# Mask tables of a block-causal attention in float32r in place of bf16

## The reference

```python
scores = scale * np.matmul(q, k.transpose(0, 1, 3, 2))
mask = block_i >= block_j            # block = position // 64
scores = np.where(mask, scores, -1000000000.0)
attn = softmax(scores)               # written out with its maximum and its sum
x = np.matmul(attn, v)               # then laid out as 2304 tokens x 512
h = x @ w_in;  x = (h * clip(h + 3, 0, 6) / 6) @ w_out       # 512 -> 2048 -> 512
h = x @ w_in2; out = (h * tanh(log1p(exp(h)))) @ w_out2      # 512 -> 2048 -> 512
```

## Time and profile before

| | |
|---|---|
| median of 3 runs | 1002.57 us (1001.17 to 1003.04) |
| profiled execution, its own time | 1002.3 us |
| span of the profiled execution | 1000.5 us |
| busy share of TensorE, VectorE, ScalarE, GpSimd | 97%, 76%, 65%, 52% |
| TensorE clock granted | full speed in all 40 slices |
| attention | from the start to about 212 us |
| masks | 128 matmuls of 64 columns, 8.9 to 206.3 us |

### The profile page before, as it was taken

How to read it: one execution, slowest core, us unless ns; L and a number is a source line. 1 busy time by engine, 2 the same in 40 slices (tenths; PEclk the granted TensorE clock), 3 DMA queues, 4 the chain that set the end, 5 groups by cost and what they waited for, 6 DMA issues and landing times.

```text
span 1000.5 us, 17885 instructions
## 1 busy us (share of the span) xinstructions
PE 966.3 (97%) x6132; PEld 857.7 (86%) x6132; DVE 764.5 (76%) x1231; ACT 645.5 (65%) x1429; POOL 523.5 (52%) x493
## 2 busy tenths in 40 slices
PE   6999999999999999999999999999999999999998
PEld 5887888899988888988888999888898988889896
DVE  5998888878687766769797776877868887776654
ACT  6888888855455444545546456777777767776663
POOL 7888899967766586957776671221212222010000
PEclk9999999999999999999999999999999999999999
DMA  6778867564689977697887455555555555465255
GB/s 159 209 190 224 225 164 203 151 183 140 221 286 321 320 259 257 205 305 265 278 270 256 168 192 183 186 194 195 189 213 193 196 202 187 168 220 197 100 182 197
DMA packets 81866, 211.49 MB, mean 211 GB/s; under 512 B 12272, under 2 KB 19056, under 8 KB 81776
## 3 DMA queue, kind: packets, MB, share of 16 engines
q1 hardware_dynamic: 81696, 210.06, 64.5%
q10 hardware_dynamic: 80, 0.29, 0.1%
HBM read 170.39 MB, written 39.92 MB: 210 GB/s over the span
## 4 chain that ended last, share of the span: by engine, by line
PE 81%; DVE 10%; issue 3%; DMA 2%; ACT 2%; POOL 1%; SPq 0%; ACTq 0%; DVEq 0%; POOLq 0%
PE psum L927 33%; PE psum L810 11%; PE psum L811 10%; PE psum L812 10%; PE psum L760 5%; PE psum L739 4%; PE psum L715 3%; PE psum L720 3%; DVE glo L1455 2%; DMA ext_d<-ext_made 2%; DVE staged L1473 2%; DVE ebuf L1449 1%; DVE ext_made L1387 1%; DVE ebuf L1468 1%; DVE ebuf L1480 1%
## 5 line engine op out<-in xcount | busy, mean ns | idle before, releaser
L927 PE MATMUL psum<-ghi,osplit 128*128 128x512 f32 (+1 forms) x640 | 215.5, 371 | 0.4 <-POOL osplit L1699 0.4
L810 PE MATMUL psum<-xhi,whi 128*128 128x256 f32 (+1 forms) x640 | 188.4, 294 | 2.0 <-ACT snap L1135 2.0
L812 PE MATMUL psum<-xhi,wlo 128*128 128x256 f32 (+1 forms) x640 | 187.7, 293 | 0.0
L811 PE MATMUL psum<-xlo,whi 128*128 128x256 f32 (+1 forms) x640 | 187.6, 293 | 0.0
L927 PE MATMUL psum<-osplit,ghi 128*128 128x512 f32 x576 | 182.0, 397 | 5.2 <-DVE glo L1455 5.2
L1455 DVE SCALAR_TENSOR_TENSOR glo<-ebuf,ghi 128x512 fp32r<-128x512 f32 x144 | 133.5, 927 | 24.4 <-ACT ghi L1183 17.3
L1686 POOL TENSOR_TENSOR xlo<-xst,xhi 128x512 fp32r<-128x512 f32 (+1 forms) x62 | 87.2, 1425 | 120.6 <-ACT xhi L1096 120.6
L1699 POOL TENSOR_TENSOR osplit<-oraw,osplit 128x512 fp32r<-128x512 f32 x80 | 117.1, 1466 | 36.4 <-ACT osplit L1102 32.3
L810 PEld LDWEIGHTS psum<-xhi,whi 128*128 128x128 f32 x640 | 121.5, 190 | 16.9 <-ACT snap L1135 5.1
L1183 ACT ACTIVATE ghi<-ebuf 128x512 fp32r<-128x512 f32 x144 | 90.3, 627 | 64.6 <-DVE ebuf L1449 34.3
L927 PEld LDWEIGHTS psum<-ghi,osplit 128*128 128x128 f32 x640 | 118.3, 189 | 15.8 <-issue 0.6
(11 more groups left out here) (102 smaller groups left out, 2294.2 us busy)
## 6 DMA issues: line engine op xcount, KB each, us to landing
ext<-ext_d SPq DMA_DIRECT2D x56, 768.0 KB, 4.4
osplit<-o_d SPq DMA_DIRECT2D x80, 512.0 KB, 5.3
oraw<-in_w_out SPq DMA_DIRECT2D x80, 256.0 KB, 5.8
qkin<-in_qk SPq DMA_DIRECT2D x63, 288.0 KB, 4.4
wraw<-in_w_in SPq DMA_DIRECT2D x32, 512.0 KB, 5.3
ext_d<-ext_made SPq DMA_DIRECT2D x32, 384.0 KB, 5.7
attn_t<-ostage SPq DMA_DIRECT2D x64, 144.0 KB, 3.1
o_d<-staged SPq DMA_DIRECT2D x32, 256.0 KB, 5.5
```

The source lines that it names most:

```text
L810: pe.matmul(dst, hi, xh, start=(start and cc == 0), stop=False, skip_group_check=True)
L811: pe.matmul(dst, hi, xl, start=False, stop=False, skip_group_check=True)
L812: last = pe.matmul(dst, lo, xh, start=False, stop=(stop and cc == 1), skip_group_check=True)
L927: last = pe.matmul(bank(Y_BANK + c, n), stat, mov, start=(first and m == 0), stop=(final and m == 2), skip_group_check=True)
```

## The change

The two tables become float32r tiles. [...] `three`, `one` and the two `negmax` tiles become slices of one tile `small`, and TensorE waits for a third signal.

```diff
-        three = sb("three", [P, 1], F32)
-        one = sb("one", [P, 1], F32)
+        small = sb("small", [P, 2 + 2 * NT], F32)
+        three, one = small[:, 0:1], small[:, 1:2]
+        negmax = [small[:, 2 + s * NT:2 + (s + 1) * NT] for s in range(2)]
         ident = sb("ident", [P, P], F32)
-        mask_rows = sb("mask_rows", [P, P], BF16)
-        mask_val = sb("mask_val", [P, DH], BF16)
-        negmax = [sb(f"negmax{s}", [P, NT], F32) for s in range(2)]
+        mask_rows = sb("mask_rows", [P, P], F32R)
+        mask_val = sb("mask_val", [P, DH], F32R)
...
-            pe.wait_ge(consts_ready, 2)
+            pe.wait_ge(consts_ready, 3)
...
+            raw_rows, raw_val = oraw[0][:, 0:P], oraw[0][:, P:P + DH]
+            nc.gpsimd.memset(raw_rows, 0.0).then_inc(memset_done, 1)
+            nc.gpsimd.memset(raw_val, MASKED).then_inc(memset_done, 1)
             nc.gpsimd.memset(ident[:, :], 0.0).then_inc(memset_done, 1)
-            nc.gpsimd.memset(mask_rows[:, :], 0.0).then_inc(memset_done, 1)
-            nc.gpsimd.memset(mask_val[:, :], MASKED).then_inc(memset_done, 1)
-            nc.gpsimd.memset(three[:, :], 3.0).then_inc(memset_done, 1)
-            nc.gpsimd.memset(one[:, :], 1.0).then_inc(memset_done, 1)
+            nc.gpsimd.memset(three, 3.0).then_inc(memset_done, 1)
+            nc.gpsimd.memset(one, 1.0).then_inc(memset_done, 1)
             pool.wait_ge(memset_done, 5)
+            nc.gpsimd.memset(raw_rows[0:1, 0:DH], 1.0).then_inc(memset_done, 1)
             nc.gpsimd.affine_select(out=ident[:, :], ...).then_inc(consts_ready, 1)
-            nc.gpsimd.memset(mask_rows[0:1, 0:DH], 1.0).then_inc(consts_ready, 1)
+            nc.gpsimd.tensor_copy(mask_val[:, :], raw_val).then_inc(consts_ready, 1)
+            pool.wait_ge(memset_done, 6)
+            nc.gpsimd.tensor_copy(mask_rows[:, :], raw_rows).then_inc(consts_ready, 1)
```

More of the change, by code:

```diff
@@ L9 @@
 F32R = mybir.dt.float32r
-BF16 = mybir.dt.bfloat16
 AX = mybir.AxisListType
```

## The result

The changed kernel is slightly faster: 1000.24 us median of 11 runs (997.41 to 1002.14), against 1002.88 us of the kernel before (11 runs, 1001.17 to 1004.66). The ratio is 0.9974 with a 95% interval of 0.9963 to 0.9985, so -2.6 us. The forecast was 1003.0 us and no change; the time lies inside the range, and the direction was missed.

A forecast was written before the change was run, and what follows sets the result against it. TensorE was taken to bound 20 of 32 heads, POOL most others; +0.05 - 3 x 0.01 = +0.02 us a head gave +0.4 us on 1002.57, so 1003.0 us, range 999.8 to 1006.2.

The forecast's parts named there:

- The mask's row: TensorE in the attention: float32r mask load pulled forward, -0.01 us in each of tiles 1 to 3, +0.05 us in tile 0.
- The 64-column matmul in float32r: Mask's matmul on TensorE in the attention: not slower than the load for klo under which it lies, 0 us.
- the constants on POOL: Start of the kernel: two added copies and a wait, hidden by the load of the first q and k, 0 us.
- The weights' fast load: Mask's weight load: by the skill page, 53 ns longer each in float32r; with nothing to hide it, 80 masks make +4.3 us.
- rival 1: L715 to L720: float32r mask load not pulled forward or delays klo's load; 0.10 us a mask, +8.2 us, chance 0.20.
- Rival 2: Mask loads in the attention: one type ends a stall from type changes; up to 0.07 us a mask, -5.6 us, chance 0.16.
- rival 3: Attention: POOL bounds more than counted, so nothing visible changes, 1002.6 us; chance 0.64 together with the forecast.
- 20 heads, with 80 of the 128 masks: Attention: heads where TensorE's own time counts; in the other 12 heads, 48 masks, small changes fall into its gaps.
- POOL's 5.36 us of 5.75: Head without extra work: POOL's busy time, cited against POOL bounding more of the attention; TensorE sets the pace.
- the moved tiles: All tiles behind the tables move by some hundred bytes: no effect assumed, counted in the range only.
- So only the first fifth of the run can change: Whole run: only the attention uses the tables, with masks between 8.9 and 206.3 us, so nothing later can change.
- time outside the attention: Sign that the prediction is wrong: a time change outside the attention, which none of the change's steps touches.

The follow-up runs named there:

- e1_types: Kernel after with its float32r tables placed inside ghi0, so every other tile lies as in the kernel before: 1.0002 against before.
- e12_no_mask: Kernel before with the mask's matmuls left out, all tiles where they were: 0.9974 (0.9958 to 0.9990) against before.
- e2_layout: Kernel before, bf16 tables, padded so every other tile lies where it does after the change (320 bytes further): 0.9981 against before.
- e5_pad64: Kernel before with all tiles behind the tables 64 bytes further: 0.9987 (0.9976 to 0.9998) against before.
- e8_pad256: Kernel before with all tiles behind the tables 256 bytes further: 1.0004 (0.9991 to 1.0017) against before.
- e11_x192_o128: Kernel before with float32r tables inside ghi0, x tiles 192 and osplit 128 bytes further modulo 256: 0.9965 against before.
- e6_pad128: Kernel before with all tiles behind the tables 128 bytes further: 1.0029 (1.0011 to 1.0047) against before.
- e7_pad192: Kernel before with all tiles behind the tables 192 bytes further: 0.9993 (0.9983 to 1.0002) against before.
- e16_all64: Kernel before with every tile 64 bytes further, all distances between tiles kept: 1.0002 (0.9986 to 1.0018) against before.
- e9_x192: Kernel before with float32r tables inside ghi0 and only the x tiles 192 bytes further modulo 256: 0.9955 (0.9939 to 0.9971) against before.

## Why the prediction was right or wrong

**The mask's row: right.** The load is pulled forward, and costs nothing in tiles 1 to 3. Medians over the heads, from the start of the `khi` matmul to the start of the one behind `klo`: 0.446 to 0.429 us in tile 1, 0.650 to 0.637 in tile 2, 0.698 to 0.680 in tile 3. For tile 0 I take the load for `khi` to the load behind `klo`, relative to the `khi` matmul: +0.035 us. Forecast were -0.01 for each of the three and +0.05. The sum for a head is -0.013 us where I had +0.02. e1_types, which is this alone, has 1.0002 (0.9992 to 1.0012), and that can't tell the forecast's +0.4 us from -0.3. The 64-column matmul in float32r doesn't lengthen these rows, and the constants on POOL are hidden, as forecast. (The prediction counts "one memset less"; there are six before and six after, and only the two copies are new.)

**The weights' fast load: the row decided.** The load's duration went from 96 to 192 ns. The Trainium skill, page "TensorE: Matmul & The Clock Gate", section "Weight-path perf modes — Fast Weight Load (FWL) and DoubleRow", gives the bf16 load about twice the speed, and the durations agree with that. The 4.3 us that the prediction estimates from it didn't come (e1_types): the load is hidden in three tiles of four, and in the fourth the row grew by 0.035 us.

**Rivals 1 to 3.** The mechanisms of rivals 1 and 2 didn't occur at their size. Rival 2 had the right sign for a wrong reason: going over to one type shortens the row by 0.013 to 0.018 us in tiles 1 to 3, not by 0.07, and lengthens it in tile 0. Its price was also too high: leaving out all masks is worth 2.6 us, so 5.6 us weren't to be had from a part of their cost. (For rival 1, a slowdown, e12_no_mask sets no such bound.) The step that failed there is "20 heads, with 80 of the 128 masks". 80 masks at the measured 0.11 us of the row would be 9 us, and 2.6 us reached the end, as the wait for POOL's `k_lo` takes 0.2 us back even in a head where TensorE is busy for 5.75 of 5.75 us. That is the mechanism of rival 3, which the prediction put aside with "POOL's 5.36 us of 5.75".

**The step that failed for the direction.** It is the sentence on the moved tiles: "No row of before tells what that costs; from the rows nothing speaks for an effect, and I count it in the range only." A term was put at nothing without a reason, and the runs show about -2 us in its place. The tiles' move by 320 bytes is the whole measurable effect: e2_layout has it without the type (-1.9 us, -3.2 to -0.6), e1_types the type without it (+0.2 us, -0.8 to +1.2), e5_pad64 has it at the same distance modulo 256, and e8_pad256 loses it. Behind it stands "So only the first fifth of the run can change": the 4704 matmuls behind the attention weren't looked at, on the ground that they use no table, and the gain lies there. It is the last of the prediction's own signs of being wrong, time outside the attention. The trace of before did show room: a matmul of 256 columns at 2.4 GHz streams for 107 ns, and they stood 119 apart. That the time still fell inside the range is luck; the range was made for the sizes of rivals that didn't occur.

**What stays open.** Shown is that spacings of TensorE's matmuls depend on the distances of tiles modulo 256 bytes, and on several tiles at once. Not shown is by what mechanism, and why the tiles of L927 and those of L810 to L812 change each other's spacing; that it happens only where the two stand near each other or x is still in use narrows it. Distances finer than 64 bytes, and the best combination, weren't tried.

## What to carry to other kernels

A change that makes a tile larger or smaller moves every tile declared behind it. Before its time is put down to what it was made for, run one kernel with the old code at the new places and one with the new code at the old places. In a kernel bound by short TensorE matmuls, a few tens of bytes between the stationary and the moving tiles are worth trying by themselves: here 192 bytes ahead of x gave 4.5 us of 1002 (2.9 to 6.1), beside the 2.6 us (1.5 to 3.7) of the change under study. The best place isn't to be worked out from one pair of tiles: e11_x192_o128 was better in one line and worse in the other. And what a whole part of the work is worth at the end is learnt by leaving it out, not by its share of a busy engine: here half of what TensorE saved in a head came back as a wait for the next engine.

## What the runs showed of the hardware

Float32r matmuls of 256 columns with a weight load each follow each other at medians of 114 to 120 ns, by where tiles lie. The class with moved weights and unmoved x has medians of 119, 114, 120, 118, 119 and 114 ns at 0, 64, 128, 192, 256 and 320 bytes (before, e5_pad64, e6_pad128, e7_pad192, e8_pad256, e2_layout). Those of 512 columns have medians of 226 to 236 ns. The pattern repeats after 256 bytes (e5_pad64 and e2_layout, e8_pad256 and before) and doesn't depend on the absolute address (e16_all64, 64 bytes). It isn't set by one matmul's own two tiles alone: L927 went from 232 to 227 ns with x at 192 (e9_x192), but its last 44 distances, far from any matmul with x, stayed at 227. A bf16 weight load between float32r ones isn't pulled under the matmul before it: in tiles 0 to 3 it starts 0.17, 0.23, 0.28 and 0.34 us behind the load for `khi`, and the float32r load that takes its place 0.11 us behind it in each (before and after).
